# TensorE's recurrence steps written out without a loop, with no-ops between some matmuls

## The chip, the cores and the metric

One core of one Trainium2 chip. The metric is the device time of one execution in microseconds, as the median of repeated runs. An engine is driven by a sequencer, which reads its program, waits for semaphores and hands matmuls and weight loads to TensorE's queue.

## The reference

Three stages follow each other. A recurrence over 768 time steps is computed for 4 x 8 heads of 48 channels: `state = w*state + k (x) v`, and `y = r . (state + u*k (x) v)`. Its output, 3072 tokens of 384 channels, goes through two MLPs of width 2048:

```python
h = x @ w_in                     # 3072x384 by 384x2048
g = where(h > 0, h, exp(min(h, 0)) - 1)
x = g @ w_out                    # the second MLP: g = h * sigmoid(1.702 * h)
```

All is float32.

## The kernel before

The recurrence is cut into 8 steps of 384 time steps, two for each batch entry (`STEPS = 8`). A step i on TensorE consists of `near(i)` (products within 32 time steps), five `level(i, k)` (products at doubling distances), `turn` (transposes), `keys_values` and `outputs`. VectorE and ScalarE assemble what comes out. The first MLP works on the same 384 tokens as a group g; while step i of the recurrence runs, group g = i - 1 of the MLP runs between its parts.

An MLP group has 16 tiles f of 128 hidden channels. `up(g, q, f)` makes hidden tile f with nine matmuls of 128x384, `down(g, f, ...)` adds it into three accumulators with nine more. The nine come from splitting each factor into a high and a low part (lo by hi, hi by hi, hi by lo) for three blocks of 128 channels. `step(b, i, half, g, q)` writes the order of all this out by hand: a unit(f) is up of tile f + 2 and down of tile f, and the recurrence's parts stand between units. The last tile of a step, unit(15), comes after `near(i + 1)`.

The order of TensorE's program is: step 0 of the recurrence alone (`first_near` to `keys_values(0, 0)`, `first_outputs`), then `up(0, 0, 0)`, `near(1)`, `up(0, 0, 1)`, `step(0, 1, ...)`; then a hardware loop over b = 1, 2 whose body is two steps (steps 2 and 3, then 4 and 5); then steps 6 and 7 written out; then the last group of the first MLP and the eight groups of the second, of which six stand in a loop of three rounds with two groups each (`group`, no recurrence).

Inside the loop the semaphore values that `up`, `down` and `level` wait for come from registers; in the written-out steps they are constants. The other engines have loops of their own over the same steps. Lines that matter below: L1288 and L1301 are the matmuls of up and down, L1020 and L1058 those of near and the levels, L1094 the last level, L1101 turn, L1136 keys_values, L1164 and L1172 outputs (from scores, from states), L1231 and L1237 the same for step 0, L1380 the loop over the steps, L1078 the wait of a level.

Of the kernel before, what the change touches and what calls it, by code (L numbers as in the profile page):

```python
# [12 lines left out]
B, H, S, D = 4, 8, 768, 48  # L13
# [8 lines left out]
KT = DM // P  # L22
NF = FF // P
WF = 2 * KT * P
GROUPS = 2 * B
STEPS = 2 * B
# [14 lines left out]

PLACE = ((0, 0), (1, 0), (0, U), (1, U), (2, 0), (2, U))

def number(g, f):
    return g * NF + f
# [12 lines left out]
def build(nc, r_dram, k_dram, w_dram, ucol_dram, v_dram, weights1, weights2, masks_dram, ident_dram, out_dram):  # L60
    x2_dram = nc.dram_tensor("x2_scratch", (KEPT, P, KT * T), F32).ap()
    with ExitStack() as ctx:
# [55 lines left out]
        def is_first(i):  # L118
            return type(i) is int and i == 0
# [4 lines left out]
        def kv_banks(i):  # L124
            return (FIRST[0], FIRST[1], FIRST[2]) if is_first(i) else BANKS
# [42 lines left out]
        def hidden(f):  # L168
            return psum[:, f % 2, 0:T]

        def acc(q, m):

            return psum[:, 2 + 3 * q + m, 0:T]
# [9 lines left out]
        def w_tile(f, lo, o):  # L183
            at = (2 * f + lo) * WF + o
            return w_split[:, at:at + P]
# [52 lines left out]
        def kv_view(i, c):  # L238

            z, slot = PLACE[c]  # L240
            return kv_banks(i)[z][:, slot * D:(slot + U) * D].rearrange("p (u e) -> p u e", u=U)

        with nc.Block() as block:
# [767 lines left out]
            def _(pe):  # L1011
# [59 lines left out]
                def level(i, k):  # L1071

                    if k < 5:
                        pe.wait_ge(pick_done, i * N_PICK + k)
                    else:
                        pe.wait_ge(pick_done, i * N_PICK + PICKS[4])
                    pe.wait_ge(upd_done, upd(i, k, 1))
                    pe.sem_inc(level_open, 1)  # L1078
                    if k == 5:
                        last_level(level_bank(i, k)).then_inc(lev_done, 2)  # L1080
                    else:
                        for pair in range(2):
                            products(1 << k, level_bank(i, k), pair).then_inc(lev_done, 1)
# [45 lines left out]
                def keys_values(i, half):  # L1129

                    def product(c, u, a):
                        z, slot = PLACE[c]
                        rows = slice(64 * (c % 2), 64 * (c % 2) + 64)
                        at = (slot + u) * D
                        n = (u * NB + c // 2) * P + 64 * a
                        return pe.matmul(kv_banks(i)[z][64 * a:64 * a + 64, at:at + D], kt[rows, n:n + 64],  # L1136
                                         v_sb[rows, c // 2, u, a, :], start=True, stop=True)

                    pe.wait_ge(v_in, i * 16 + 16)
                    pe.wait_ge(kt_done, i * N_KT + N_KT)  # L1140
                    if is_first(i):
                        pe.wait_ge(pick_done, PICKS[1])
                    pe.sem_inc(level_open, 1)
                    for n, (even, odd) in enumerate(((4, 1), (0, 3), (2, 5))):
                        if n == 2 and half == 0:
                            pe.wait_ge(kv_done, i * N_KV + 1)
                            pe.sem_inc(level_open, 1)
                        for u in range(U):
                            for a in range(2):
                                mm = product(even, u, a)  # L1150
                                if odd < 5 or half == 0:
                                    mm = product(odd, u, a)
                        mm.then_inc(kv_done, 1)
# [66 lines left out]
                def first_outputs():  # L1220

                    def place(c, u, a):
                        z, slot = PLACE[c]
                        to = 64 * (a ^ (u % 2))
                        if u == U - 1:
                            return FIRST[6 + c % 2][to:to + D, c // 2 * CH:(c // 2 + 1) * CH]
                        return y_banks(0)[z][to:to + D, (slot + u) * CH:(slot + u + 1) * CH]
# [41 lines left out]
                                            mm = from_state(c, uu, a)  # L1269
                        mm.then_inc(y_done, 2 if n == 2 else 1)  # L1270

                def up(g, q, f, second=False):

                    if type(g) is int and g == 0:
                        pe.wait_ge(wlo_done, f + 1)
                    if second:
                        pe.wait_ge(w2lo_done, f + 1)
                    if type(g) is not int or g > 0 or f > 1:
                        pe.wait_ge(gate_done, number(g, f - 1))
                    n = 0  # L1280
                    for m in range(KT):
                        if f == 0 and is_first(g):
                            pe.wait_ge(xlo_first, m + 1)
                        elif f == 0:
                            pe.wait_ge(xlo_done, g * KT - KT + m + 1)
                        xh, xl = x_hi[q][:, m * T:(m + 1) * T], x_lo[q][:, m * T:(m + 1) * T]
                        for lo, xx in ((0, xl), (0, xh), (1, xh)):
                            mm = pe.matmul(hidden(f), w_tile(f, lo, m * P), xx, start=n == 0, stop=n == 3 * KT - 1)  # L1288
                            n += 1
                    mm.then_inc(h_done, 1)  # L1290

                def down(g, f, to, freed=False, last=False):

                    if freed:
                        pe.wait_ge(acc_act, g)
                        pe.wait_ge(acc_dve, g * 2)
                    pe.wait_ge(lo_done, number(g, f + 1))
                    gh, gl = g_hi[:, f % 4, :], g_lo[:, f % 4, :]
                    for m in range(KT):
                        for n, (lo, gg) in enumerate(((0, gl), (0, gh), (1, gh))):  # L1300
                            mm = pe.matmul(acc(to, m), w_tile(f, lo, (KT + m) * P), gg,  # L1301
                                           start=f == 0 and n == 0, stop=f == NF - 1 and n == 2)
                        if last:
                            mm.then_inc(last_acc, 1)
                    if not last:
                        mm.then_inc(l2_done, 1)

                def step(b, i, half, g, q, more=True, s=0):

                    def unit_up(f):  # L1310
                        if f + 2 < NF:
                            up(g, q, f + 2)
                        else:
                            up(g + 1, 1 - q, f + 2 - NF)

                    def unit_down(f):
                        down(g, f, 0, freed=f == 0 and (type(g) is not int or g > 0))

                    def unit(f):
                        unit_up(f)  # L1320
                        unit_down(f)

                    for f in range(s):
                        unit(f)
                    unit_up(s)
                    level(i, 1)
                    unit_down(s)
                    unit(1 + s)
                    level(i, 2)
                    unit(2 + s)  # L1330
                    unit_up(3 + s)
                    level(i, 3)
                    unit_down(3 + s)
                    unit(4 + s)
                    level(i, 4)
                    unit(5 + s)
                    unit_up(6 + s)
                    level(i, 5)
                    unit_down(6 + s)
                    unit(7 + s)  # L1340
                    turn(i)
                    unit(8 + s)
                    unit_up(9 + s)
                    keys_values(i, half)
                    unit_down(9 + s)
                    unit(10 + s)
                    unit_up(11 + s)
                    outputs(b, i, half)
                    unit_down(11 + s)
                    for f in range(12 + s, 15):  # L1350
                        unit(f)
                    if more:
                        near(i + 1)
                    unit(15)
# [17 lines left out]
                first_turn(0)  # L1372
                first_turn(1)
                keys_values(0, 0)
                first_outputs()
                up(0, 0, 0)
                near(1)
                up(0, 0, 1)
                step(0, 1, 1, 0, 0)
                with pe.Fori(1, B - 1) as b:  # L1380
                    step(b, b * 2, 0, b * 2 - 1, 1)
                    step(b, b * 2 + 1, 1, b * 2, 0)
                step(B - 1, STEPS - 2, 0, STEPS - 3, 1)
                step(B - 1, STEPS - 1, 1, STEPS - 2, 0, more=False)
                group(KEPT, 1)
                with pe.Fori(0, PAIRS - 1) as b:
                    for q in range(2):
# [61 lines left out]
```

## Time and profile before

| | us |
|---|---|
| median of 3 runs (976.7 to 979.65) | 976.77 |
| the profiled execution | 978.74 |
| its span | 976.9 |
| TensorE busy (matmul) | 937.8 |
| VectorE busy | 546.7 |
| ScalarE busy | 456.1 |

The profiled execution took 1.8 us more than its span, the part of it in which instructions of the kernel ran. Until 48 us step 0 runs, to 509 us the steps with the first MLP between them, and after that the MLP groups alone. The mean granted TensorE clock is 0.986 of full speed.

### The profile page before, as it was taken

What the parts mean: (1) busy time and instruction counts of PE and PEld (TensorE: products, weight loads), DVE (VectorE), ACT (ScalarE), POOL (GpSimd) and SP (SyncE); (2) the same over time, 40 slices, a digit from 0 to 9 for tenths busy, and PEclk for the clock granted to TensorE, in tenths of its full rate; (3) what the DMA queues carried; (4) which work ended last, traced back from release to release, by engine and by line L of the source; (5) the groups of instructions that cost most, each with busy time, mean ns of one, the idle gap of its engine ahead of it and who ended that gap; (6) DMA issues with size and microseconds to landing.
All of it is one profiled execution on the core that took longest, in us unless ns stands there. A gap on an engine that the chain in (4) does not pass through costs nothing.

```text
span 976.9 us, 27105 instructions
## 1 busy us (share of the span) xinstructions
PE 937.8 (96%) x11872; PEld 912.9 (93%) x11872; DVE 546.7 (56%) x915; ACT 456.1 (47%) x874; POOL 67.6 (7%) x81
## 2 busy tenths in 40 slices
PE   4589999999999999999999999999999999999998
PEld 4479999999899899999999999999999999999998
DVE  8878686685675766866844444343433344333333
ACT  2547637546456355374455764333333333333332
POOL 1261000000000000000000641000000000000000
PEclk8799999999999999999999999999999999999999
DMA  6443211211402212113005510000000000000000
GB/s 186 106 137 91 57 52 26 65 44 28 105 3 56 76 26 56 52 25 82 3 7 201 201 53 1 25 1 24 0 25 0 24 0 20 4 1 25 1 25 25
DMA packets 15798, 47.30 MB, mean 48 GB/s; under 512 B 2864, under 2 KB 6832, under 8 KB 15696
## 3 DMA queue, kind: packets, MB, share of 16 engines
q1 hardware_dynamic: 13680, 40.85, 14.9%
q0 software_dynamic: 1536, 4.50, 1.6%
q8 instruction: 87, 1.43, 0.7%
q10 hardware_dynamic: 480, 0.40, 0.2%
q14 instruction: 15, 0.12, 0.0%
HBM read 35.71 MB, written 8.85 MB: 46 GB/s over the span
## 4 chain that ended last, share of the span: by engine, by line
PE 95%; issue 2%; DVE 2%; DMA 1%; ACT 0%; ACTq 0%; DVEq 0%
PE psum L1288 42%; PE psum L1301 42%; PE psum L1058 4%; PE psum L1020 1%; PE psum L1172 1%; PE psum L1136 1%; PE psum L1164 1%; PE psum L1101 1%; PE psum L1094 1%; DVE arena L708 0%; DVE blocks L762 0%; DMA x_raw<-y 0%; DMA arena<-k_channels_dram 0%; DVE arena L702 0%; PE psum L1067 0%
## 5 line engine op out<-in xcount | busy, mean ns | idle before, releaser
L1288 PE MATMUL psum<-x_hi,w_split 128*128 128x384 f32 x1536 | 395.6, 338 | 2.7 <-issue 2.7
L1301 PE MATMUL psum<-g_hi,w_split 128*128 128x384 f32 x1536 | 392.0, 336 | 0.0
L1288 PEld LDWEIGHTS psum<-x_hi,w_split 128*128 128x128 f32 x1536 | 281.4, 189 | 3.6 <-issue 3.6
L1301 PEld LDWEIGHTS psum<-g_hi,w_split 128*128 128x128 f32 x1536 | 277.6, 188 | 0.0
L1288 PE MATMUL psum<-x_lo,w_split 128*128 128x384 f32 x768 | 263.9, 344 | 5.9 <-DVE x_lo L799 4.4
L1301 PE MATMUL psum<-g_lo,w_split 128*128 128x384 f32 x768 | 261.6, 341 | 0.2 <-issue 0.2
L507 ACT ACTIVATE g_hi<-gate 128x384 fp32r<-128x384 f32 x256 | 134.5, 525 | 170.6 <-DVE gate L818 88.1
L823 DVE TENSOR_TENSOR g_lo<-gate,g_hi 128x384 fp32r<-128x384 f32 x256 | 143.6, 561 | 118.3 <-ACT g_hi L507 118.3
L816 DVE TENSOR_TENSOR gate<-expo,psum 128x384 f32<-128x384 f32 x128 | 70.8, 553 | 162.6 <-ACT expo L503 162.6
L1288 PEld LDWEIGHTS psum<-x_lo,w_split 128*128 128x128 f32 x768 | 144.6, 188 | 7.9 <-issue 7.0
L1301 PEld LDWEIGHTS psum<-g_lo,w_split 128*128 128x128 f32 x768 | 144.5, 188 | 3.0 <-issue 0.7
L503 ACT ACTIVATE expo<-psum 128x384 f32<-128x384 f32 x128 | 63.0, 492 | 172.7 <-PE psum L1288 172.7
L818 DVE SCALAR_TENSOR_TENSOR gate<-expo,psum 128x384 f32<-128x384 f32 x128 | 71.1, 555 | 119.4 <-ACT expo L498 119.1
L496 ACT ACTIVATE expo<-psum 128x384 f32<-128x384 f32 x128 | 62.5, 488 | 131.0 <-PE psum L1288 130.7
L702 DVE TENSOR_TENSOR arena<-arena 128x1536 f32<-128x1536 f32 (+1 forms) x54 | 85.3, 1580 | 5.3 <-PE psum L1058 4.4
L498 ACT ACTIVATE expo<-expo 128x384 f32<-128x384 f32 x128 | 67.3, 526 | 4.0
L1058 PEld LDWEIGHTS psum<-arena 128*32 128x32 f32 (+1 forms) x3840 | 41.5, 111 | 16.7 <-issue 9.9
L1058 PE MATMUL psum<-arena 128*32 128x32 f32 (+1 forms) x3840 | 46.8, 203 | 8.4 <-DVE arena L708 5.8
L708 DVE TENSOR_TENSOR arena<-arena 128x768 f32<-128x768 f32 (+1 forms) x54 | 46.6, 862 | 0.0
L376 POOL DMA_DIRECT2D x_raw<-y x21 | 10.1, 486 | 411.7 <-ACT x_raw L468 215.6
L762 DVE COPY_PREDICATED blocks<-masks,psum 128x384 f32<-128x384 int32 x40 | 30.5, 762 | 2.0 <-DVE blocks L762 1.6
L448 ACT ACTIVATE blocks<-blocks 32x768 f32<-32x768 f32 x31 | 26.0, 840 | 3.4 <-DVE blocks L762 2.9
(94 smaller groups left out, 449.2 us busy)
## 6 DMA issues: line engine op xcount, KB each, us to landing
v_sb<-v_tokens_dram SPq DMA_DIRECT2D x8, 576.0 KB, 5.7
arena<-w_channels_dram SPq DMA_DIRECT2D x14, 288.0 KB, 5.0
arena<-k_channels_dram SPq DMA_DIRECT2D x14, 288.0 KB, 4.4
arena<-r_channels_dram SPq DMA_DIRECT2D x14, 288.0 KB, 4.6
x_scratch<-x_sb SPq DMA_DIRECT2D x7, 576.0 KB, 3.3
arena<-x_scratch SPq DMA_DIRECT2D x1, 4032.0 KB, 12.8
staging<-weights_dram SPq DMA_DIRECT2D x9, 384.0 KB, 3.6
blocks<-weights_dram SPq DMA_DIRECT2D x9, 384.0 KB, 3.7
```

Source lines behind the costliest of these rows:

```text
L496: act.activation(expo[:, f % 2, :], hidden(f), ACT.Relu, scale=-1.0).then_inc(neg_done, 1)
L498: act.activation(expo[:, f % 2, :], expo[:, f % 2, :], ACT.Exp, scale=-1.0).then_inc(exp_done, 1)
L503: act.activation(expo[:, f % 2, :], hidden(f), ACT.Sigmoid, scale=1.702).then_inc(exp_done, 1)
L507: act.activation(g_hi[:, f % 4, :], gate[:, f % 2, :], ACT.Copy).then_inc(hi_done, 1)
L702: return dve.tensor_tensor(z, z, by, ALU.mult)
L708: return dve.tensor_tensor(z, z, d[:, :, 1:2].to_broadcast([P, d.shape[1], h]), ALU.mult)
L816: dve.tensor_tensor(gate[:, f % 2, :], expo[:, f % 2, :], hidden(f), ALU.mult).then_inc(gate_done, 1)
L818: dve.scalar_tensor_tensor(out=gate[:, f % 2, :], in0=expo[:, f % 2, :], scalar=-1.0, in1=hidden(f), op0=ALU.add, op1=ALU.max).then_inc(ga ...
L823: dve.tensor_tensor(g_lo[:, f % 4, :], gate[:, f % 2, :], g_hi[:, f % 4, :].bitcast(F32), ALU.subtract).then_inc(lo_done, 1)
L1058: mm = pe.matmul(bank[32 * j:32 * j + n, at:at + 32].rearrange("p (a b h) -> p a b h", a=2, h=h), kk[:, u, o:o + n], r[:, :, u, o:o + 32]. ...
L1288: mm = pe.matmul(hidden(f), w_tile(f, lo, m * P), xx, start=n == 0, stop=n == 3 * KT - 1)
L1301: mm = pe.matmul(acc(to, m), w_tile(f, lo, (KT + m) * P), gg, start=f == 0 and n == 0, stop=f == NF - 1 and n == 2)
```

## The change

TensorE's program alone is changed. The loop over b = 1, 2 is replaced by a Python loop that writes steps 2 to 7 out, with constants for all waits. Two runs of no-ops, 116 and 120, are put ahead of and behind `first_outputs`. In certain tiles of the MLP, 15 or 25 no-ops are spread behind the nine matmuls by `fill_of`: 25 gives 2 or 3 behind each. `FILL[i]` names the tiles: for steps 2 to 7 both halves of unit(15) (which stands behind near(i)), unit(0) and unit(1), 150 no-ops in all; for step 1 eight tiles from unit(7) on, 160 in all. The tiles of the last step's unit(15) have none.

```diff
+FIRST_FILL = (116, 120)
+FILL = {i: {("up", 15): 25, ("down", 15): 25, ("up", 0): 25, ("down", 0): 25, ("up", 1): 25, ("down", 1): 25}
+        for i in range(2, 2 * 4)}
+FILL[1] = {("up", 7): 15, ("down", 7): 15, ("up", 8): 15, ("down", 8): 15, ("down", 9): 25, ("up", 10): 25, ("down", 10): 25,
+           ("up", 11): 25}
+
+
+def fill_of(i, kind, f, n):
+
+    count = FILL.get(i, {}).get((kind, f), 0)
+    return count * (n + 1) // 9 - count * n // 9
...
+                def fill(count):
+
+                    for _ in range(count):
+                        pe.nop(hint="fill")
...
                             mm = pe.matmul(hidden(f), w_tile(f, lo, m * P), xx, start=n == 0, stop=n == 3 * KT - 1)
+                            if filled and n < 3 * KT - 1:
+                                fill(fill_of(*filled, n))
                             n += 1
                     mm.then_inc(h_done, 1)
+                    if filled:
+                        fill(fill_of(*filled, n - 1))
...
+                            if filled and 3 * m + n < 3 * KT - 1:
+                                fill(fill_of(*filled, 3 * m + n))
...
                     def unit_up(f):
+                        filled = (i + 1 if f == 15 else i, "up", f)
...
+                        down(g, f, 0, freed=f == 0 and g > 0, filled=(i + 1 if f == 15 else i, "down", f))
...
                 keys_values(0, 0)
+                fill(FIRST_FILL[0])
                 first_outputs()
+                fill(FIRST_FILL[1])
                 up(0, 0, 0)
                 near(1)
                 up(0, 0, 1)
                 step(0, 1, 1, 0, 0)
-                with pe.Fori(1, B - 1) as b:
-                    step(b, b * 2, 0, b * 2 - 1, 1)
-                    step(b, b * 2 + 1, 1, b * 2, 0)
-                step(B - 1, STEPS - 2, 0, STEPS - 3, 1)
-                step(B - 1, STEPS - 1, 1, STEPS - 2, 0, more=False)
+                for i in range(2, STEPS):
+                    step(i // 2, i, i % 2, i - 1, (i - 1) % 2, more=i < STEPS - 1)
```

## Rows read from the trace of the kernel before

**Rows 1.** The page: busy time and share of each engine; the chain by engine.

```profile
PE 937.8 (96%) x11872; PEld 912.9 (93%) x11872; DVE 546.7 (56%) x915; ACT 456.1 (47%) x874; POOL 67.6 (7%) x81
...
PE 95%; issue 2%; DVE 2%; DMA 1%; ACT 0%; ACTq 0%; DVEq 0%
```

**Rows 2.** Timeline of TensorE, 453 to 460.9 (near(7)): start, length, instructions, [idle before].

```profile
453.14 0.88 PE L1020 MATMUL psum<-arena 128*32 128x64 f32 x48
...
455.44 0.44 PE L1288 MATMUL psum<-x_lo,w_split 128*128 128x384 f32 x1
455.72 0.51 PE L1288 MATMUL psum<-x_hi,w_split 128*128 128x384 f32 x2
...
456.24 0.51 PE L1288 MATMUL psum<-x_hi,w_split 128*128 128x384 f32 x2
...
457.45 0.45 PE L1301 MATMUL psum<-g_lo,w_split 128*128 128x384 f32 x1 [0.18 <-issue]
```

**Rows 3.** TensorE's waits, 52 to 513: us in total, times, longest.

```profile
PE psum L1288 <- issue: 4.2, 6, 1.7
PE psum L1172 <- issue: 3.8, 4, 1.3
PE psum L1058 <- issue: 2.6, 4, 0.9
```

**Rows 4.** DMA queues, 566 to 654 (MLP only): packets, MB, share.

```profile
q8 instruction: 5, 0.08, 0.4%
```

**Rows 5.** All DMA queues there are from 664 to 874 (inside the last loop).

```profile
q1 hardware_dynamic: 1600, 2.36, 3.1%
q14 instruction: 2, 0.02, 0.0%
```

**Rows 6.** Timeline of TensorE behind near(1).

```profile
54.31 0.34 PE L1288 MATMUL psum<-x_lo,w_split 128*128 128x384 f32 x1
56.32 0.62 PE L1288 MATMUL psum<-x_hi,w_split 128*128 128x384 f32 x2 [1.68 <-issue]
```

**Rows 7.** Timeline of TensorE in outputs of step 1.

```profile
107.59 0.61 PE L1172 MATMUL psum<-arena,state 48*48 48x64 f32 x22 [1.08 <-issue]
```

**Rows 8.** Timeline of TensorE behind near(3).

```profile
188.77 0.34 PE L1288 MATMUL psum<-x_hi,w_split 128*128 128x384 f32 x1
189.56 0.45 PE L1288 MATMUL psum<-x_hi,w_split 128*128 128x384 f32 x1 [0.45 <-issue]
```

**Rows 9.** Stretches of outputs: length, busy PE PEld DVE ACT POOL, clock, DMA.

```profile
103.91:108.53 4.62, 3.54 (x194) 3.22 (x193) 3.74 (x9) 3.14 (x7) 0.00 (x0) 1.00 0.02 4
...
504.11:508.94 4.83, 3.55 (x193) 3.23 (x193) 1.11 (x2) 1.54 (x3) 0.00 (x0) 1.00 0.01 3
```

**Rows 10.** The same view behind outputs of step 7, TensorE alone.

```profile
509.25:512.45 3.20, 3.20 (x11) 0.50 0.12 28
```

**Rows 11.** Timeline of TensorE where the loop over the steps jumps back.

```profile
257.37 0.51 PE L1301 MATMUL psum<-g_hi,w_split 128*128 128x384 f32 x2
259.03 0.44 PE L1288 MATMUL psum<-x_lo,w_split 128*128 128x384 f32 x1 [1.15 <-issue]
...
262.39 0.51 PE L1058 MATMUL psum<-arena 128*32 128x32 f32 x36 [0.92 <-issue]
```

**Rows 12.** TensorE's sequencer by line: ns min/median/max, first and last start us.

```profile
L1380 PEldq COMPARE_BRANCH  x2: 83/2166/4248, 254.6 to 390.6; - x2
...
L1026 PEldq FUSED_REGOPS  x1: 37/37/37, 384.5 to 384.5; - x1
...
L1032 PEldq ALU_OP  x1: 36/36/36, 384.8 to 384.8; - x1
```

**Rows 13.** Timeline of TensorE, 33.5 to 48.5, around first_outputs.

```profile
38.03 2.78 PE L1231 MATMUL psum<-blocks,v_sb 64*48 64x64 f32 x96 [3.77 <-ACT blocks L448]
...
47.89 0.66 PE L1288 MATMUL psum<-x_lo,w_split 128*128 128x384 f32 x1 [4.43 <-DVE x_lo L799]
```

**Rows 14.** The sequencer's wait ahead of level 1 of step 7, as rows 12.

```profile
L1078 PEldq EVENT_SEMAPHORE  x1: 2335/2335/2335, 457.5 to 457.5; - x1
```

More of the change, by code:

```diff
@@ L1270, in first_outputs, with up @@
                         mm.then_inc(y_done, 2 if n == 2 else 1)
-                def up(g, q, f, second=False):
+                def fill(count):
+                    for _ in range(count):
+                        pe.nop(hint="fill")
+                def up(g, q, f, second=False, filled=None):
                     if type(g) is int and g == 0:
@@ L1288, in up, with down @@
                             mm = pe.matmul(hidden(f), w_tile(f, lo, m * P), xx, start=n == 0, stop=n == 3 * KT - 1)
+                            if filled and n < 3 * KT - 1:
+                                fill(fill_of(*filled, n))
                             n += 1
                     mm.then_inc(h_done, 1)
-                def down(g, f, to, freed=False, last=False):
+                    if filled:
+                        fill(fill_of(*filled, n - 1))
+                def down(g, f, to, freed=False, last=False, filled=None):
                     if freed:
@@ L1306, in down @@
                         mm.then_inc(l2_done, 1)
+                    if filled:
+                        fill(fill_of(*filled, 3 * KT - 1))
                 def step(b, i, half, g, q, more=True, s=0):
                     def unit_up(f):
+                        filled = (i + 1 if f == 15 else i, "up", f)
                         if f + 2 < NF:
-                            up(g, q, f + 2)
+                            up(g, q, f + 2, filled=filled)
                         else:
-                            up(g + 1, 1 - q, f + 2 - NF)
+                            up(g + 1, 1 - q, f + 2 - NF, filled=filled)
                     def unit_down(f):
-                        down(g, f, 0, freed=f == 0 and (type(g) is not int or g > 0))
+                        down(g, f, 0, freed=f == 0 and g > 0, filled=(i + 1 if f == 15 else i, "down", f))
                     def unit(f):
```

## The prediction

> **What bounds the kernel now.** First the page's busy table and chain [rows 1]: TensorE is busy for 96% of the span and carries 95% of the chain that ended last, nearly all of it in the two MLP lines. So what can be gained is time in which TensorE has work and does not do it. Next the timeline around near(7) gives the paces [rows 2]: three MLP matmuls start within 455.72 to 456.24, 0.175 us each, 1.57 us for a tile of nine; the change from small matmuls to an MLP tile takes 0.28.
>
> The list of TensorE's waits over the steps [rows 3] names "issue" almost alone: 11.0 us with two more lines of 0.2, in which nothing that the profile shows is missing (1.5 us of L1058's 2.6 are step 1's levels 2 and 3, which wait for VectorE). Modelled ends overlap, so behind an MLP matmul the true loss is 0.17 us more than the row says.
>
> What one costs: near(i) and outputs() are runs of 384 and 352 or 384 small instructions. In near(7), from 453.14 to 455.44 [rows 2], a block end lies by the count 147 instructions in, at about 454.0; TensorE stands at the next one, 256 further, until 457.45. In near(3) it is 144 in (about 185.95), and TensorE goes on at 189.56 [rows 8]. So the next block is there 3.5 to 3.6 us after the last was entered, and one that is used up sooner stalls.
>
> By the Trainium skill (Runtime: NRT & Kernel Launch, section Instruction fetch mechanics) blocks are 256 instructions and crossing one is "mostly hidden". [Rows 4] agree with the size, [rows 6 to 8] not with hidden; where it held, only the loop's part below would be gained.
>
> **What is removed**, start to start:
> - Behind near(1): 54.31 to 56.32, where 0.17 is due: 1.84 us [rows 6].
> - outputs() of steps 1, 3, 5, 7: they span 4.62, 4.06, 4.39 and 4.83 us with 3.54, 3.52, 3.51 and 3.55 busy (four rows, the first and the last in [rows 9]): 1.08 + 0.54 + 0.88 + 1.28 = 3.78.
> - After the last of these the granted clock is 0.50 for 3.2 us (1.2 GHz, else 2.4), and 11 matmuls take 0.32 us instead of 0.175 [rows 10]: 1.6.
> - Behind near(3): 188.77 to 189.56 less 0.175 is 0.61 [rows 8]; near(7) 0.34 (0.18 idle + 0.17) [rows 2]; near(5) and (6) by the same reading 0.73 and 0.41. Sum 2.1.
> - The loop: one COMPARE_BRANCH takes 4248 ns, where it jumps back [rows 12]. TensorE, with a filled queue, loses 1.15 idle + 0.17 = 1.32, then 1.10 in the level behind it (start to start, around the 0.92 idle) [rows 11], 0.37 in the next, and twice 0.32 behind level 1 of steps 3 and 5, at ends that move too. Sum 3.4.
>
> All: 12.7 us. By the same page of the skill a taken branch to a block that is not held waits for its fetch; the 4248 ns agree.
>
> **Where the ends come to lie.** A written-out step is 2392 instructions and 17 waits that stand alone; with 6 x 25 no-ops 2559, ten blocks less one, so the ends stand nearly still from step to step. With 236 no-ops ahead of near(1) and 160 in step 1, an end lies 142 in first_outputs, 156 in near(1), 160 in outputs(1), 152 to 157 in near(2) to near(7), and 160 or 127 in the later outputs. A run of 384 always holds one; the second falls behind it. That ends the stalls in outputs(): 230 instructions at 3.5/390 us, then 26 of MLP, are 4.3 us, over 3.6. Behind near(1) it is 4 us: also covered.
>
> Not so behind near(2) to near(7): the second end is 24 instructions behind the run, and in that very tile the 25 no-ops make that five matmuls. TensorE gets there 2.58 us (run and turn, 453.14 to 455.72 [rows 2]) + 0.87 = 3.45 after the run's start; the block comes at 0.87 + 3.6 = 4.45. I expect a new stall of 1.0 us in each of six steps: **+6.0**. Bounds: 0 (if the queue's lead over TensorE covers it) and 1.2 x 6 = 7.2.
>
> **The no-ops themselves**, 1296. The trace has none. Below: a weight load or small matmul passes in 2.3/384 us = 6 ns [rows 2], and nothing is saved by one, so not under zero. Above: the register operations of TensorE's queue take 36 to 37 ns themselves but start 0.1 us apart (four in a row, the first and last in [rows 12]). I take 40 ns, near the operation's own time, since a no-op has no operand; both ends are kept.
>
> By the skill's some 20 cycles an instruction (the same section; the sequencer's 1.2 GHz: Advanced Engine Details and Errata, Clock Domains), an estimate of 17 ns, all of them would be covered; no row here shows it.
> - 116 stand ahead of first_outputs, beside 3.77 us of idle in which TensorE waits for ScalarE [rows 13], 3.99 from the last start before it. 116 x 0.04 = 4.64: 0.65 late, and on the path, since x and the first MLP tile follow from first_outputs.
> - 120 stand behind it, beside the 4.43 (4.64) us in which x_lo is made [rows 13]: 4.8, 0.16 late. With a little lead of the sequencer both together cost +0.7.
> - 25 in a tile: 1.0 + 18 x 0.006 = 1.1 us of issue beside 1.57 of matmul: hidden up to 59 ns. Queued behind them are the rest of the tile and, three tiles on, level 1's wait: in step 7 the sequencer stands there from 457.5 for 2.3 us [rows 14], which ends 0.9 ahead of TensorE's first matmul of the level; 75 no-ops are 3.0 us and use up that lead, no more.
>
> Sum: -12.7 + 6.0 + 0.7 = **-6.0 us**. The profiled execution took 978.74 (span 976.9, 1.8 around it), the median is 976.77: 972.7 profiled, **970.8** as a median. Changes under 0.3% (2.9 us) count as none.
>
> **Rivals.**
> 1. No stall behind near(2) to near(7): -12.0, 964.8. For it: near(2) now has an end 36 in and shows no stall, since the sequencer crossed it early. Against: 152 is beyond that lead, and 147 did stall.
> 2. The other side: slow no-ops. From 59 ns on they outlast their tile: 36 tiles x (25c + 0.1 - 1.57), and the first 236 cost 236c - 8.6. Break-even with the 6.7 of the rest is at c = 60 ns. At 65 ns it is 5.6 + 6.7 - 6.7 = +5.6, 982; at the 0.1 us of [rows 12] 37 + 15 - 6.7 = +45, 1022. For it: those rows; against: they are operations with operands.
> 3. The no-ops occupy nothing (merged away). Steps are then 2409 long and the ends wander by 151: by the count, stalls behind near(1), near(4), near(6) and in outputs of steps 1, 3, 5, 6 sum to 9.4 us, so 12.7 - 9.4 = 3.3 is gained, 973.5.
> 4. TensorE comes earlier and waits for VectorE: level 1's data was only 0.9 us ahead of it in step 7 [rows 14]. If over half of the gain is given back, 974.
>
> **Chances.** Forecast 0.47 (own range 966.5 to 974: no-ops of 20 to 53 ns, near stalls 3 to 7 us), rival 1 0.12, rival 2 0.22, rival 3 0.09, rival 4 0.10. Faster by over 0.3% (under 973.9): 0.42 + 0.12 + 0.05 + 0.03 = 0.62; within: 0.05 of the forecast, 0.04 of rival 3, 0.07 of rival 4 and 0.04 of the low end of rival 2 = 0.20; slower 0.18. Range 964 to 982: below lies 0.04, above 0.13 of rival 2.
>
> **What would show it.** Right: no idle over 0.5 us in L1172; clock 1.0 at 509; no gap at 257; L1288 gaps near 1 us half a tile behind near(2) to near(7); the gaps before 38 and 47.9 grown by 0.7 together. Wrong: MLP tiles with no-ops over 1.6 us, or a first MLP matmul after 49.5 (rival 2); near gaps absent (1); outputs gaps that stay (3); waits for VectorE at the levels (4).

## The result and the profile after

The changed kernel takes 998.78 us in the median (996.89 to 999.93, five runs) beside 976.77 of the kernel before: a ratio of 1.021 (95% interval 1.020 to 1.023), so it is 22 us slower. The forecast was 970.8, faster. The profiled execution has a span of 998.1 us against 976.9: 21.2 us to explain.

TensorE's waits for "issue" (nothing that the profile shows is missing) over the whole span: us in total, times, longest. [Rows 3] have the steps of before alone.

```profile
PE psum L1308 <- issue: 13.2, 7, 8.6
PE psum L1246 <- issue: 8.0, 1, 8.0
...
PE psum L1073 <- issue: 5.2, 4, 2.8
```

L1308 is the matmul of up, L1246 the first of first_outputs, L1073 that of the products in near and the levels, L1325 that of down. The line of outputs(), 3.8 us in [rows 3], is gone. In its place stand two single waits of over 8 us; the other 4.5 us of L1308 are six waits behind near(2) to near(7). The timeline around first_outputs says where, and what was there before stands in [rows 13]:

```profile
47.21 2.81 PE L1246 MATMUL psum<-blocks,v_sb 64*48 64x64 f32 x96 [8.01 <-issue]
...
61.01 0.66 PE L1308 MATMUL psum<-x_lo,w_split 128*128 128x384 f32 x1 [8.61 <-issue]
```

Both idles were 3.77 and 4.43 us and had a releaser on another engine; now they are about twice as long and have none. TensorE's sequencer shows who holds it. Its no-ops by window, from 38, 50 and 411.3 us (ns min/median/max, first and last start):

```profile
L1290 PEldq NOP  x116: 13/13/13, 38.4 to 47.0; - x116
...
L1290 PEldq NOP  x120: 13/13/13, 51.8 to 60.8; - x120
...
L1290 PEldq NOP  x25: 13/13/13, 411.4 to 413.4; - x25
```

A no-op's record is 13 ns long, yet 116 of them fill 8.6 us and 120 fill 9.0. In an unbroken row most starts are 71 ns apart (669 of the 1295 distances are exactly 71), and every 11 to 16 no-ops one distance is longer, 0.10 to 0.23 us. The mean over both rows is 75 ns.

In the tiles the 25 last 2.0 us by themselves; where a pair of weight load and matmul stands between two no-ops their starts are 91 ns apart, 20 more. So a tile with them takes 25 x 0.071 + 9 x 0.020 = 1.96 us, or 2.06 with the mean of 75 ns, where the matmuls alone need 1.57. One such tile, as a stretch (length, busy PE, clock, DMA):

```profile
207.62:209.80 2.18, 2.18 (x11) 1.00 0.01 4
```

It appears as busy, since a matmul's modelled length covers the longer distance: the page's busy TensorE time grew from 937.8 to 952.0 us, and "busy" hides the loss.

The stretch of outputs in step 7 and what follows, which answers to [rows 9] and [rows 10]:

```profile
528.47:531.68 3.21, 3.21 (x194) 1.00 0.02 5
528.47:536.00 7.53, 7.53 (x218) 1.00 0.11 24
```

There is no stall inside, and the granted clock stays at 1.00 (2.4 GHz). And behind near(2), in the first tile with no-ops:

```profile
134.69 0.33 PE L1308 MATMUL psum<-x_hi,w_split 128*128 128x384 f32 x1
135.78 0.34 PE L1308 MATMUL psum<-x_hi,w_split 128*128 128x384 f32 x1 [0.76 <-issue]
```

135.78 is the sixth matmul of the tile: it stands after five, 1.09 us start to start.

### The profile page after: what moved, and what is told of

Read it like the earlier page. It is cut to its first block, busy times and chain, and to the rows that moved or that the text cites. A ratio compares the mean times of both kernels' runs of the same rounds, so it can differ in the third digit from the quotient of the medians.

```text
span 998.1 us, 28228 instructions
## 1 busy us (share of the span) xinstructions
PE 952.0 (95%) x11872; PEld 914.6 (92%) x11872; DVE 547.4 (55%) x915; ACT 457.2 (46%) x874; POOL 67.6 (7%) x81
## 4 chain that ended last, share of the span: by engine, by line
PE 94%; issue 3%; DVE 1%; DMA 1%; ACT 0%; SPq 0%; POOL 0%; DVEq 0%; ACTq 0%; POOLq 0%
PE psum L1308 42%; PE psum L1325 42%; PE psum L1073 4%; PE psum L1035 1%; PE psum L1187 1%; PE psum L1151 1%; PE psum L1179 1%; PE psum L1116 1%; PE psum L1109 1%; DMA arena<-k_channels_dram 1%; DMA x_raw<-y 0%; DVE blocks L777 0%; DVE arena L723 0%; PE psum L1082 0%; PE psum L1246 0%
## 5 line engine op out<-in xcount | busy, mean ns | idle before, releaser
L1308 PE MATMUL psum<-x_hi,w_split 128*128 128x384 f32 x1536 | 399.1, 340 | 0.8 <-issue 0.8
L1325 PE MATMUL psum<-g_hi,w_split 128*128 128x384 f32 x1536 | 396.5, 339 | 0.0
L1308 PEld LDWEIGHTS psum<-x_hi,w_split 128*128 128x128 f32 x1536 | 281.3, 188 | 4.8 <-issue 1.0
L1325 PEld LDWEIGHTS psum<-g_hi,w_split 128*128 128x128 f32 x1536 | 277.2, 188 | 5.1 <-issue 0.4
L1308 PE MATMUL psum<-x_lo,w_split 128*128 128x384 f32 x768 | 266.4, 347 | 12.4 <-issue 12.4
L1325 PE MATMUL psum<-g_lo,w_split 128*128 128x384 f32 x768 | 263.8, 343 | 0.0
L1308 PEld LDWEIGHTS psum<-x_lo,w_split 128*128 128x128 f32 x768 | 144.4, 188 | 17.9 <-issue 14.3
L1325 PEld LDWEIGHTS psum<-g_lo,w_split 128*128 128x128 f32 x768 | 144.1, 188 | 5.2 <-issue 0.4
L1073 PEld LDWEIGHTS psum<-arena 128*32 128x32 f32 (+1 forms) x3840 | 41.7, 112 | 17.7 <-issue 12.1
L1073 PE MATMUL psum<-arena 128*32 128x32 f32 (+1 forms) x3840 | 46.8, 203 | 10.2 <-issue 5.2
L723 DVE TENSOR_TENSOR arena<-arena 128x768 f32<-128x768 f32 (+1 forms) x54 | 46.6, 863 | 0.0
```

The costliest lines, as they stand in the source:

```text
L723: return dve.tensor_tensor(z, z, d[:, :, 1:2].to_broadcast([P, d.shape[1], h]), ALU.mult)
L1073: mm = pe.matmul(bank[32 * j:32 * j + n, at:at + 32].rearrange("p (a b h) -> p a b h", a=2, h=h), kk[:, u, o:o + n], r[:, :, u, o:o + 32]. ...
```

## The experiments

All kernels are the changed one with other numbers or places of no-ops; `...` marks what is left out of a diff. Times are medians; a ratio is to the kernel before, timed beside the run, with its 95% interval. A block end is the place where one block of 256 instructions ends and the next begins.

**x1_plain**: written out, no no-op.

```diff
-FIRST_FILL = (116, 120)
-FILL = {...}
+FIRST_FILL = (0, 0)
+FILL = {}
```

> TensorE's steps written out, no no-op at all. Theory N (the no-ops are the loss: the sequencer passes one in 71 ns, so 25 in a tile last longer than its matmuls): the loss goes, the loop's stalls (3.4 us) and the half clock at 509 (1.6 us) go as well, block ends lie wherever they fall: 973.5 us by my earlier count (971 to 976), first MLP matmul near 48 us. Theory W (the written-out program itself is what costs, by its longer code and more fetches): still slower than before by 10 us or more, 987 or above.

Measured: 976.21 us beside 977.15 of before, ratio 0.9997 (0.9984 to 1.0009). Theory W falls: the written-out program costs nothing. The 973.5 was too low. In its profile the loop's stalls are gone, but block ends fall at new places, and TensorE still waits for "issue" over the steps:

```profile
PE psum L1305 <- issue: 3.3, 2, 1.9
PE psum L1070 <- issue: 3.0, 3, 1.5
PE psum L1184 <- issue: 2.2, 2, 1.3
```

(up, products, outputs from states; 1.5 of the 3.0 us are in near, the rest in two levels of step 1, another 1.1 us are in near on a line of their own, and 1.1 wait for VectorE.) From the first MLP matmul to the second tile behind the last outputs it needs 460.7 us in its profile against 465.9 before, but its step 0 is 1.4 us longer, and the timed runs show no difference.

**x3_block**: the same numbers of no-ops, each tile's in one run behind its last matmul (up is shown, down likewise).

```diff
                             mm = pe.matmul(hidden(f), ...)
-                            if filled and n < 3 * KT - 1:
-                                fill(fill_of(*filled, n))
...
                     if filled:
-                        fill(fill_of(*filled, n - 1))
+                        fill(FILL.get(filled[0], {}).get(filled[1:], 0))
```

> The changed kernel with the same no-ops, each tile's 25 or 15 in one run behind its last matmul instead of spread between the nine. Theory N with the pace read from the trace (71 ns a no-op, about 20 ns more for each matmul pair that stands between two of them): a tile with 25 takes 1.78 + 0.11 = 1.9 us instead of 2.1, 40 tiles give 8 us back, and the stall behind near(2) to near(7) shrinks since nine matmuls instead of five stand ahead of the block end (some 4 us): 985 to 991. Theory S (only the number of no-ops counts, not where they stand): 998 to 999.

Measured: 995.52 us, ratio 1.020 (1.0175 to 1.0225), outside both ranges: a miss. A tile with 25 does shrink, to 1.86 to 2.07 us, but the tile behind near grows from 2.6 to 3.0 us to 3.1 to 3.7. Timeline behind near(2):

```profile
134.80 0.41 PE L1323 MATMUL psum<-g_lo,w_split 128*128 128x384 f32 x1 [1.82 <-issue]
```

The nine matmuls do stand ahead of the block end, but only six of their no-ops do (131.0 to 131.4 us). The other 19 start from 133.29 on, once the block is there, and are then paid in full: 1.5 us until the next matmul at 134.80, with nothing left for TensorE to do. I had counted the matmuls that come ahead, not the no-ops left behind.

**x4_nofirst**: no no-ops at first_outputs.

```diff
-FIRST_FILL = (116, 120)
+FIRST_FILL = (0, 0)
...
-FILL[1] = {..., ("down", 9): 25, ("up", 10): 25, ("down", 10): 25, ("up", 11): 25}
+FILL[1] = {..., ("down", 9): 17, ("up", 10): 17, ("down", 10): 16, ("up", 11): 16}
```

> The changed kernel without the 236 no-ops around first_outputs, and with 126 instead of 160 in step 1, so that a block end lies 166 in near(2) and later ones (152 before). Theory N: the 8.5 us at first_outputs go, 1.8 us of stall behind near(1) come back, the later near stalls lose 0.35 us each: 988 to 992, and first_outputs begins 3.8 to 4.2 us after the last matmul of keys_values. Rival F (those two gaps grew because step 0 was late anyway, 4.9 us already ahead of the first no-op): gaps of 8 us stay, 996 to 999.

Measured: 985.31 us, ratio 1.009 (1.006 to 1.011), 13.5 under the changed kernel and also under the 988 to 992 expected. Rival F falls; both gaps are nearly back at their length and have their releasers again:

```profile
40.83 2.81 PE L1246 MATMUL psum<-blocks,v_sb 64*48 64x64 f32 x96 [3.95 <-ACT blocks L463]
...
50.91 0.66 PE L1308 MATMUL psum<-x_lo,w_split 128*128 128x384 f32 x1 [4.79 <-DVE x_lo L814]
```

The two gaps together are 8.0 us shorter than in the changed kernel (8.5 are between that and before). Another 2.2 us is step 0 ahead of them, which ends earlier in this profile; theory N had not counted it. The kernel still is slower than before, and the tiles do it: those of steps 2 to 7 take 319.7 us in sum against 305.3.

**x5_spread**: as many no-ops as x4_nofirst, at most 15 in a tile, none right behind near.

```diff
-FILL = {i: {("up", 15): 25, ("down", 15): 25, ("up", 0): 25, ("down", 0): 25, ("up", 1): 25, ("down", 1): 25}
-        for i in range(2, 2 * 4)}
+FILL = {i: {(kind, f): 15 for kind in ("up", "down") for f in (2, 4, 5, 7, 8)} for i in range(2, 2 * 4)}
+FILL[1] = {(kind, f): 14 for kind in ("up", "down") for f in (2, 4, 5, 7)} | {("up", 8): 14}
```

> Written out, no no-ops at first_outputs, 126 in step 1 and 150 in each later step as before, but 14 or 15 in a tile and only in tiles between near and outputs that are not behind near; block ends lie 166 in near and 174 or 141 in outputs. Theory N with a threshold of 19 no-ops in a tile (19 x 71 + 9 x 20 ns = 1.53 us): all no-ops hidden, tiles 1.57 us, no stall behind near(2) to near(7), none in outputs: 12.7 - 1.8 = 10.9 us under before, 964 to 968. Rival P (each no-op takes its 20 ns of TensorE wherever it stands, as 0.5 us in a tile of 25): 1026 x 0.02 = +20.5, so 985 to 988.

Measured: 967.59 us (966.28 to 968.24), ratio 0.991 (0.989 to 0.994). The same kernel again, on the chip of the runs that follow:

> x5_spread once more, beside x6_shift and x7_early: 967 to 968 again. The time until the last matmul of keys_values(0, 0) was 34.0 to 38.9 us in five profiles of the same program text: I expect another value in that band here, unrelated to the kernel.

Measured: 964.95 us beside 978.76 of before, ratio 0.986 (0.985 to 0.988). That is 2 us under what was expected, while before was at 978.76 there. This version beats the kernel before by about 1% and the changed one by about 3%. All 1026 no-ops are hidden: the MLP tiles of steps 2 to 7 take 300.8 us in sum, as without any (300.6 in x1_plain); rival P falls. TensorE's waits from 56 to 510 us, nearly all of steps 1 to 7:

```profile
PE psum L1323 <- issue: 0.8, 1, 0.8
PE psum L1071 <- issue: 0.7, 1, 0.7
PE psum L1306 <- issue: 0.5, 1, 0.5
```

Only the last is a block end, behind near(1). The first two are in step 1 and end 0.1 us after a VectorE operation that TensorE needs, as two of [rows 3]'s do.

**x6_shift**: x5_spread with 96 more no-ops in step 1, so that all later block ends lie elsewhere.

```diff
-FILL[1] = {(kind, f): 14 for kind in ("up", "down") for f in (2, 4, 5, 7)} | {("up", 8): 14}
+FILL[1] = {(kind, f): 15 for kind in ("up", "down") for f in (2, 4, 5, 7, 8, 9, 10)} | {("up", 11): 12}
```

> x5_spread with 96 more no-ops in step 1, all in tiles of 15 or fewer, so that a block end lies 70 (not 166) in near(2) to near(7) and 78 or 45 in outputs; everything else as in x5_spread. Theory B (a block used up within 3.6 us of its start stalls): the second end now lies inside the run as well, near stalls by 3.6 - 1.5 = 2.1 us six times, outputs by about 1.3 us seven times: 21 us over x5_spread, some half clock with it: 987 to 992. Rival H (crossing a block end is mostly hidden, and x5_spread gained by something else, such as more lead of the sequencer): within 2 us of x5_spread, 966 to 970.

Measured: 986.98 us, ratio to before 1.010 (1.008 to 1.012), 22.0 over x5_again. Rival H falls. In the two profiles, 20.7 us apart, near(2) to near(7) take 10.7 us more and the seven outputs 7.9 us more: 18.6 us for where the ends lie. The rest is nearly all step 0, which ends 1.9 us later and varies from profile to profile (last part of the next section). Its waits from 58 us to the end of the steps:

```profile
PE psum L1071 <- issue: 10.3, 7, 1.9
PE psum L1185 <- issue: 6.1, 7, 1.2
```

These are six in near, the one VectorE wait in step 1 that x5_again has too, and seven in outputs. In near(3) of x6_shift TensorE stops with 29 of 192 matmuls to go, so 163 matmuls or 326 instructions in: 70 + 256, where the count puts the second end. All six in near come after 163 to 165 matmuls.

```profile
194.45 0.45 PE L1071 MATMUL psum<-arena 128*32 128x32 f32 x29 [1.44 <-issue]
```

**x2_dose**: x1_plain with growing numbers of no-ops in the tiles of the last group of the first MLP.

```diff
+FILL = {99: {("dose", f): (5, 10, 15, 20, 25, 30, 40, 0)[f // 2] for f in range(16)}}
...
+                def dose(g, f):
+
+                    return (99, "dose", f) if type(g) is int and g == KEPT else None
...
-                        down(g, f, q, last=tail and f == NF - 1)
+                        down(g, f, q, last=tail and f == NF - 1, filled=dose(g, f))
```

> x1_plain with 5, 10, 15, 20, 25, 30 and 40 no-ops in the tiles of the last group of the first MLP (four tiles of each number, nothing but MLP matmuls around them). Theory N with a queue: the sequencer needs 0.071 n + 0.18 us a tile, TensorE 1.57, and TensorE eats up a lead of at most 64 queued instructions (5.6 us) before it feels the difference: tiles with up to 25 stay at 1.57 here, those with 30 may, those with 40 take 3.0 us at the end. Rival P (a tile of 25 takes 2.1 us wherever it stands): 2.1 already here, 2.45 with 30.

One run, 982.58 us. The four tiles each with 25, 30 and 40 as stretches, and the sequencer's no-ops of the first tile with 25:

```profile
544.25:550.53 6.28, 6.28 (x38) 1.00 0.37 109
550.53:559.73 9.20, 9.20 (x37) 1.00 0.46 130
559.73:572.46 12.73, 12.52 (x37) 1.00 0.23 72
...
L1287 PEldq NOP  x25: 13/13/13, 542.0 to 543.9; - x25
```

A tile takes 1.57 us with 25, as with 20 and fewer; 2.30 with 30 (2.03 in the first, 2.4 in the others); 3.18 with 40. So 25 cost nothing as long as the sequencer has a lead, but they use it up. From the tiles with 5 to the first with 20, a tile's first no-op starts 2.8 us before TensorE reaches the tile, half of the 5.6 that I had allowed for; at the first tile with 25 it is 2.3 us (542.0 against 544.25), at the first with 30 0.35, at the first with 40 nothing. The sequencer needs 2.05 us for a tile with 25, so a fifth such tile would not have been free. The same 25 cost 0.5 us behind near, where 384 small instructions have used the lead up (0.2 us behind near(3) of the changed kernel). Rival P falls again. With the mean of 75 ns, 0.075 n + 0.18 gives 2.43 and 3.18 us for 30 and 40, about what the tiles without a lead take. By it, an estimate, 18 no-ops a tile could be kept up without end, not 19.

**x7_early**: x5_spread plus the 236, placed in waits of step 0.

```diff
-FIRST_FILL = (0, 0)
+FIRST_FILL = (50, 50)
...
                 def first_level(k, pair):
 
+                    fill((0, 6, 6, 6, 5, 5)[k])
...
+                fill(80)
                 pe.wait_ge(cleared_p, 3)
```

> x5_spread with the 236 no-ops that the first part lacks, put where the sequencer waits anyway: 80 at its start, 56 over the waits of step 0's levels, 50 ahead of and 50 behind first_outputs (3.6 us each, beside gaps of 3.7 and 4.4 us). Block ends lie 156 in near(1), 186 or more in the later ones. Theory N: all hidden, the 1.8 us behind near(1) gained: 965 to 967. Rival Q (in step 0 the no-ops add up on the path, as 8.5 us did around first_outputs): up to 236 x 0.071 = 17 us more, 970 to 984.

Measured: 967.06 us (965.70 to 969.20), ratio to before 0.989 (0.9875 to 0.991), beside 0.986 (0.985 to 0.988) of x5_again. In its profile near(1) and the tile behind it no longer stall (3.98 us together instead of 6.01 in x5_again), but first_outputs begins 4.0 us after keys_values instead of 2.5, and the first MLP tile 5.6 us after first_outputs instead of 3.5. It lies at the upper edge of theory N and brings no gain; if anything it is 2 us slower than x5_again.

## Why the prediction was wrong

**The no-op's price** is the step that failed. It was taken as 40 ns, with bounds of 0 and 0.1 us, because the register operations' own records are 36 ns long [rows 12]. With it fell the overlap that the forecast built on, that 25 in a tile and the 236 at first_outputs are nearly covered. But the record is not the cost: those rows start 0.1 us apart, and the no-op, 13 ns by its record, 71 to 75. The terms of the sum then read (us):

| term | forecast | measured |
|---|---|---|
| stalls, loop and half clock removed | -12.7 | -15.4 (remainder) |
| new stalls behind near(2) to near(7) | +6.0 | +4.5 |
| 36 tiles with 25 no-ops in steps 2 to 7 | 0 | +17.1 |
| four such tiles in step 1 | 0 | +1.6 |
| 236 no-ops at first_outputs | +0.7 | +8.5 |
| step 0 ahead of the first no-op | 0 | +4.9 |

The last column is from start distances of the profiles. first_outputs begins 8.31 us after the last start of keys_values (3.99 before), the first MLP matmul 8.83 after the last of first_outputs (4.64). The MLP tiles of steps 2 to 7 take 21.6 us more than in x5_again; of these the stalled tiles, 2.57 to 3.02 us instead of the 2.1 of their neighbours, make 4.5. What is removed is the remainder to 21.2. x5_again agrees with it: its steps take 13.7 us less than before (452.2 against 465.9), and up to outputs(1), where it keeps the stall behind near(1), 1.5 more than the changed kernel.

A second step failed beside it: step 0 ahead of the first no-op was put at nothing, and it is 4.9 of the 21.2 us. Its cause is open (below).

**What bounds and what is removed** held. Block ends of 256 instructions stall a run that holds two of them: shown by x6_shift, where only their places differ and 13 stalls come, six in near and seven in outputs. By the count TensorE goes on 2.9 to 3.6 us after it reached the block's start there; the forecast took 3.5 to 3.6, and 2.1 and 1.3 us a stall were expected where 1.8 and 1.1 came. The Trainium skill's "mostly hidden" (Runtime: NRT & Kernel Launch, Instruction fetch mechanics) agrees with the MLP stretches alone; the 18.6 us of x6_shift stand against it. outputs of steps 1, 3, 5, 7 went from 4.62, 4.06, 4.39 and 4.83 to 3.21 or 3.22 us each, and no half clock follows step 7. That is 5.0 us where the forecast had 3.8: it took their busy time of 3.5 us for what they need without the stall, and they need 3.2. x1_plain adds that removing the loop without steering the ends brings nothing that can be timed.

**Where the ends come to lie** held to a matmul: the stall behind near(2) is after five matmuls of the tile, those behind near(3) to near(7) after six. From start to start it is 0.91 us there and 0.7 to 1.0 in the others, for a forecast of 1.0; over what the no-ops of the tile cost anyway, 0.5 to 0.9 are left, 4.5 in all instead of 6.0. The first rival, that it is absent, falls.

**The hidden fill** held in kind: x5_spread's 15 a tile cost nothing. The threshold that I gave, 59 ns for 25, is near the truth and, at 71 to 75 ns, decided against the kernel.

**Rival 2** was the case, and its chance of 0.22 too low: [rows 12] held the only starts of operations that the sequencer itself carries out, and I took the value away from them. At 71 ns its formula gives about 989, since it had 12 ns and not 20 for a matmul pair and nothing for step 1's tiles and step 0. The Trainium skill's figure (Runtime: NRT & Kernel Launch, Instruction fetch mechanics), some 20 cycles an instruction, is an estimate of 17 ns with the 1.2 GHz of Advanced Engine Details and Errata, Clock Domains; for a no-op the trace has four times that. Rival 3 falls, since the no-ops stand in the trace, 1296 of them. Rival 4 holds in step 1 alone: there the waits ahead of two levels, which end with a VectorE operation 0.1 us earlier (L723 at 76.95 and 83.61 us), are 1.4 and 0.7 us in the changed kernel and 0.8 and 0.7 before. So 0.6 us of what is gained behind near(1) goes to VectorE; in steps 2 to 7 neither the changed kernel nor x5_again waits for it.

**The range** ended at 982 because the slow case was cut at 65 ns; with 0.1 us as a bound named in the text it should have reached to where that led.

What stays open is step 0. The last matmul of keys_values(0, 0) starts at 34.0 us in the profile of before and at 38.9 after, in program text that is alike, and at 34.5 to 38.8 in the others. The longest stop in it that has no releaser is this:

```profile
24.92 0.93 PE L1073 MATMUL psum<-arena 128*16 128x32 f32 x50 [2.83 <-issue]
```

The instruction queue has a transfer under way at 22.5 us, so a block that comes late is a likely cause of this stop; that is argued, not shown. Seven of the other nine profiles stop behind the same matmul, the 478th of the program, for 1.3 to 2.5 us from start to start (3.1 here); before and x7_early do not. It makes at most 2.4 of the 4.9 us. Each kernel has one or two profiles, so whether the change lengthens step 0 or these runs happened to be at the long end is not shown, nor was it tried.

## What to carry to other kernels

An instruction that the sequencer itself executes costs its start distance, not the length of its record, and padding is free only where the sequencer is ahead of its engine or waits anyway, and it uses that lead up; price it from starts, and keep it out of the tiles behind a dense run. Block ends can be worth steering: of a run of more than 256 short instructions only one end should lie inside. With runs of 352 or 384, ends between 127 and 174 instructions in did that here, and ends at 45 to 78 did not. When two rows bound an unknown cost, ask which of them is the same kind of thing.

## What was not expected of the hardware

- A no-op on TensorE's sequencer: 71 ns from start to start, 75 in the mean, 13 ns in the record; 0.08 us each in a tile of nine matmul pairs (3.18 us with 40, x2_dose).
- The sequencer's lead over TensorE pays for such instructions: 2.8 us was the most seen, and with 2.3 us of it 25 a tile were free for four tiles (x2_dose); without it they cost 0.5 us a tile.
- The position of block ends alone costs 18.6 us in 13 stretches of near and outputs (x5_again to x6_shift, 964.95 to 986.98 us in all), with no instruction of its work changed.
